# Blank TensorE products at the start of an attention and feed-forward kernel, and another order of its first loads

## The reference

```python
B, H, S, D = 4, 8, 576, 64
q_rot, k_rot = rotate(q), rotate(k)            # x1*cos - x2*sin, x1*sin + x2*cos on the halves of D
scores = matmul(q_rot, k_rot^T) / sqrt(D)      # per batch and head, 576 x 576
attn = exp(scores - max) / (sum + 1e-9)
x = (attn @ v), heads side by side             # 2304 tokens x 512
h = x @ w_in                                   # 2304 x 2048
g = max(h, 0) + alpha * min(h, 0)
out = g @ w_out                                # 2304 x 512
```

## Time and profile before

| | us |
|---|---|
| median of 3 runs | 696.17 |
| the profiled execution, whole | 695.67 |
| its span, first to last instruction | 693.9 |
| TensorE busy (PE) | 676.6 (98%) |
| VectorE busy | 369.5 (53%) |
| ScalarE busy | 316.6 (46%) |
| GpSimd busy | 281.9 (41%) |
| one queue's transfers, share of 16 DMA engines | 29.2% |

### The profile page before, as it was taken

One profiled execution on the slowest core, in us unless ns is written; L12 is line 12 of the kernel. 1 busy time (PEld: TensorE's weight loads), 2 busy tenths in 40 slices (PEclk: granted clock), 3 DMA queues, 4 the chain that ended last, 5 costly groups with the idle time before them and its releaser, 6 DMA issues.

```text
span 693.9 us, 12120 instructions
## 1 busy us (share of the span) xinstructions
PE 676.6 (98%) x4100; PEld 588.2 (85%) x4100; DVE 369.5 (53%) x681; ACT 316.6 (46%) x746; POOL 281.9 (41%) x260
## 2 busy tenths in 40 slices
PE   3899999999999999999999999999999999999998
PEld 3788888888888887698889999999999999999996
DVE  4688888888888887545642333333224322333222
ACT  2777777777777776433333222322222232223223
POOL 6655777777776503222222222222222222222222
PEclk9999999999999999999999999999999999999999
DMA  6898655666666643600001000000000000001001
GB/s 159 219 223 204 146 136 137 139 143 142 143 142 145 144 109 100 243 1 1 0 1 46 0 1 16 32 0 1 21 24 0 0 30 15 0 0 46 1 1 46
DMA packets 76619, 51.30 MB, mean 74 GB/s; under 512 B 61088, under 2 KB 61472, under 8 KB 76064
## 3 DMA queue, kind: packets, MB, share of 16 engines
q1 hardware_dynamic: 76576, 50.76, 29.2%
HBM read 22.95 MB, written 4.72 MB: 40 GB/s over the span
## 4 chain that ended last, share of the span: by engine, by line
PE 95%; DVE 2%; SPq 1%; DMA 1%; issue 0%; ACT 0%; POOL 0%; DVEq 0%
PE banks L635 29%; PE banks L664 29%; PE banks L559 14%; PE banks L517 11%; PE banks L581 10%; PE banks L577 2%; DMA k_two<-k_hi 1%; SPq L306 0%; DVE nmax L875 0%; DMA raw_q<-in_q 0%; SPq L307 0%; DVE pt L924 0%; SPq L291 0%; DVE prob L1044 0%; SPq L309 0%
## 5 line engine op out<-in xcount | busy, mean ns | idle before, releaser
L461 POOL TENSOR_TENSOR g_lo<-g,g_hi 128x384 fp32r<-128x384 f32 (+1 forms) x98 | 99.8, 1018 | 308.9 <-ACT g_hi L825 305.6
L990 DVE TENSOR_SCALAR g<-banks,alpha_sb 128x384 f32<-128x384 f32 (+1 forms) x98 | 59.8, 610 | 250.9 <-ACT pos L816 250.9
L635 PE MATMUL banks<-x_hi,w_in_lo 128*128 128x384 f32 x384 | 129.3, 337 | 0.0
L635 PE MATMUL banks<-x_hi,w_in_hi 128*128 128x384 f32 x384 | 129.2, 337 | 0.0
L635 PE MATMUL banks<-x_lo,w_in_hi 128*128 128x384 f32 x384 | 129.0, 336 | 0.0
L816 ACT ACTIVATE pos<-banks 128x384 f32<-128x384 f32 x96 | 47.1, 491 | 170.2 <-PE banks L635 170.2
L875 DVE TENSOR_REDUCE nmax<-banks 128x1 f32<-128x576 f32 x144 | 108.6, 755 | 25.2 <-PE banks L517 19.8
L664 PE MATMUL banks<-w_out_hi,g_hi 128*128 128x512 f32 x288 | 114.8, 399 | 0.3
L664 PE MATMUL banks<-w_out_hi,g_lo 128*128 128x512 f32 x288 | 112.9, 392 | 0.0
L664 PE MATMUL banks<-w_out_lo,g_hi 128*128 128x512 f32 x288 | 111.9, 389 | 0.0
L825 ACT ACTIVATE g_hi<-g 128x384 fp32r<-128x384 f32 (+1 forms) x98 | 50.9, 519 | 116.0 <-DVE g L993 116.0
(11 more groups left out here) (85 smaller groups left out, 907.4 us busy)
## 6 DMA issues: line engine op xcount, KB each, us to landing
k_two<-k_hi SPq DMA_DIRECT2D x64, 160.0 KB, 2.9
out<-stage SPq DMA_DIRECT2D x18, 256.0 KB, 2.0
raw_q<-in_q SPq DMA_DIRECT2D x32, 128.0 KB, 2.7
raw_k<-in_k SPq DMA_DIRECT2D x32, 128.0 KB, 2.4
q_two<-q_hi SPq DMA_DIRECT2D x32, 128.0 KB, 2.3
q_two<-q_lo SPq DMA_DIRECT2D x32, 128.0 KB, 2.3
q_own<-q_hi SPq DMA_DIRECT2D x32, 128.0 KB, 2.4
raw_v<-in_v SPq DMA_DIRECT2D x32, 128.0 KB, 2.3
```

What stands on the lines that cost most here:

```text
L461: nc.gpsimd.tensor_tensor(g_lo[f % 2][:, part], g[f % 2][:, part], g_hi[f % 2][:, part].bitcast(F32), ALU.subtract).then_inc(g_lo_done, 1)
L635: mm = nc.tensor.matmul(h_ps[f % 2], w[:, j, cols], xx[:, j, :], start=(step == 0), stop=(step == 3 * CT - 1))
L990: nc.vector.tensor_scalar(g[f % 2][:, part], h_ps[f % 2][:, part], 0.0, alpha_sb[:, f:f + 1], ALU.min, ALU.mult).then_inc(neg_done, 1)
```

## The change

- A new zeroed tile `blank` (128 x 128, float32), filled by VectorE, and `run_in(count)`: `count` products of `blank` with itself into PSUM bank 7, whose results nothing reads.
- 16 of these before the first transposes on TensorE, 4 between the transposes of q and of k of pair 0, 6 behind the last of them, and one ahead of each of the tiles 2 to 8 of period 0.
- `FIRST_TILES` holds tile 3 too, which then takes six products on 64 rows; tile 4 is the first that waits for the stacks. The high part of the next q waits for tile 3's products.
- ScalarE's queue issues the sin table and two of the four copies of the first k stack; the SyncE queue keeps the other two.
- In period 0 the order of SyncE's issues becomes: raw q of pair 2, q stack and k stack of pair 1, v of pair 0, raw k of pair 2.
- In period 0 the transposes of `U_K` and `U_MIXED` move behind tile 5's products; ScalarE takes tile 4's exponential ahead of the high parts of k, VectorE tile 5's maximum ahead of the low parts.
- VectorE and ScalarE wait for fewer of GpSimd's zero fills at the start.

```diff
-FIRST_TILES = (1, 2)
+FIRST_TILES = (1, 2, 3)
...
-            sp.dma_start(sin_sb[:, :, :], sin).then_inc(sin_in, 16)
             load(0, 0)
...
             stack(0, 0, 0)
-            stack(0, 0, 1)
+            sp.wait_ge(evac[U_K % T_BANKS], evac_count(-1, U_K))
+            sp.wait_ge(evac[U_MIXED % T_BANKS], evac_count(-1, U_MIXED))
+            for head, own in ((0, slice(0, D)), (1, slice(D, P))):
+                sp.dma_start(k_two[0][own, head, :].bitcast(F32), k_hi[0][own, :].bitcast(F32)).then_inc(k_two_in, 16)
...
                     if has_pair(p + 2):
                         load(p + 2, 0)
-                    load_v(b, t)
-                    if has_pair(p + 2):
+                    if not is_opening(p):
+                        load_v(b, t)
+                    if has_pair(p + 2) and not is_opening(p):
                         load(p + 2, 1)
                     if has_pair(p + 1):
                         stack(p + 1, (t + 1) % 2, 0)
                         stack(p + 1, (t + 1) % 2, 1)
+                    if is_opening(p):
+                        load_v(b, t)
+                        load(p + 2, 1)
...
+            def run_in(count):
+
+                for _ in range(count):
+                    nc.tensor.matmul(banks[:, 7, 0:P], blank[:, :], blank[:, :], start=True, stop=True)
+
             def score(p, t, n):
 
                 if not has_now(p):
                     return
+                if is_opening(p) and n > 1:
+                    run_in(1)
...
                 score(p, t, A_TILES[2])
-                turn(p, t, U_K)
-                turn(p, t, U_MIXED)
+                if not is_opening(p):
+                    turn(p, t, U_K)
+                    turn(p, t, U_MIXED)
...
                 score(p, t, B_TILES[0])
+                if is_opening(p):
+                    turn(p, t, U_K)
+                    turn(p, t, U_MIXED)
...
+            pe.wait_ge(blank_done, 1)
+            run_in(16)
             pe.wait_ge(ident_in, 16)
-            for u in (*OF_NEXT, U_MIXED):
-                turn(-1, -1, u)
+            turn(-1, -1, U_Q)
+            run_in(4)
+            turn(-1, -1, U_K)
+            turn(-1, -1, U_MIXED)
+            run_in(6)
...
+                    if isinstance(p, int) and p == 0:
+                        act.wait_ge(scored, FIRST_TILES[-1] + 1)
...
                 exps(p, t, A_TILES[2])
+                if is_opening(p):
+                    exps(p, t, A_TILES[3])
                 hi(p, U_K, t)
                 hi(p, U_MIXED, t)
-                exps(p, t, A_TILES[3])
+                if not is_opening(p):
+                    exps(p, t, A_TILES[3])
...
-            act.wait_ge(padded, PADDED)
+            act.dma_start(sin_sb[:, :, :], sin).then_inc(sin_in, 16)
+            act.wait_ge(padded, 4)
...
+            for own, head, other in ((slice(0, D), 0, slice(D, P)), (slice(D, P), 1, slice(0, D))):
+                act.dma_start(k_two[0][other, head, :].bitcast(F32), k_hi[0][own, :].bitcast(F32)).then_inc(k_two_in, 16)
...
+                if is_opening(p):
+                    maxima(p, t, B_TILES[0])
                 lo(p, U_K, t)
                 lo(p, U_MIXED, t)
...
-            nc.vector.memset(zero[:, :], 0.0).then_inc(padded, 1)
-            dve.wait_ge(padded, PADDED)
+            nc.vector.memset(blank[:, :], 0.0).then_inc(blank_done, 1)
+            nc.vector.memset(zero[:, :], 0.0).then_inc(blank_done, 1)
+            dve.wait_ge(padded, 2)
```

More of the change, by code:

```diff
@@ L50, in build @@
     PERIODS = NB * PAIRS
-    PADDED = 15
+    PADDED = 14
     W_COLS = F // (2 * PAIRS)
@@ L174, in build @@
             zero = sb(att, "zero", [P, 1])
+            blank = sb(att, "blank", [P, P])
         attention_bytes, used[0] = used[0], 0
@@ L220, in build @@
         first_step = sem("first_step")
+        blank_done = sem("blank_done")
         q_two_in, k_two_in = sem("q_two_in"), sem("k_two_in")
@@ L266, in chunks, with is_opening @@
             chunk(NCHUNK // 2 - 1, 1)
+        def is_opening(p):
+            return isinstance(p, int) and p == 0
         def is_first(i, c):
@@ L426, in _ @@
             pool.wait_ge(padded, PADDED)
+            pool.wait_ge(blank_done, 2)
             pool.wait_ge(sin_in, 16)
@@ L843, in _ @@
                 hi(-1, u, -1)
+            act.wait_ge(evac[U_K % T_BANKS], evac_count(-1, U_K))
+            act.wait_ge(evac[U_MIXED % T_BANKS], evac_count(-1, U_MIXED))
+            for own, head, other in ((slice(0, D), 0, slice(D, P)), (slice(D, P), 1, slice(0, D))):
+                act.dma_start(k_two[0][other, head, :].bitcast(F32), k_hi[0][own, :].bitcast(F32)).then_inc(k_two_in, 16)
             def batch(b):
@@ L1021, in period @@
                         split_x(0, 0, j)
-                maxima(p, t, B_TILES[0])
+                if not is_opening(p):
+                    maxima(p, t, B_TILES[0])
                 maxima(p, t, B_TILES[1])
```

## The result

The changed kernel takes 699.56 us (median of 5 runs, 698.65 to 701.77), the kernel before 696.17 (5 runs, 695.79 to 696.30): a ratio of 1.0060, 95% interval 1.0049 to 1.0071. It is slower by 3.4 us. The profiled execution took 701.77, with a span of 700.0 against 693.9.

A forecast was written before the change was run, and what follows sets the result against it. TensorE's order and waits bound the kernel, dense from 46 us. Transposes of k in period 1 move from 35.92 to 36.6, +0.7 us, kept to the end: median 696.17 becomes 696.9, range 695.2 to 700.4.

The forecast's parts named there:

- the rival with the fallen clock: Period 1, TensorE's new stall: clock falls to the low rate, 3 us lost over the 0.7, 699.9 us; chance 0.28.
- Part 1: Kernel start: raw q comes about 0.4 us earlier without the sin table on SyncE's queue; tile 0 starts 0.9 us earlier.
- Part 2: Blanks at the start and in period 0: 0.24 to 0.48 us each at the low rate, cost counted zero, clock likely raised.
- Part 4: Period 0, second k stack: issued at once when low parts of k are done at 23.15, landing at 28.1, not 31.90.
- Part 3: Period 0, tile 4: starts when the first k stack lands, taken as 18.5 us, between 17.75 and 19.0.
- E: Period 0: time when the second pair's high and low parts of k are done, 18.5 + 4.66 = 23.15 us.
- Part 5: Raw k of pair 2 behind stacks and v: rotated 13.44 us after the low parts, at 36.6; TensorE stands 4.5 us.
- The faster case: Period 1: raw k of pair 2 lands early, stall overrated, worth 3.8 us at best; chance 0.14.

The follow-up runs named there:

- The first k stack by SyncE alone: Changed kernel with raw k of pair 2 ahead of the stacks, all four first k stack copies back on SyncE's queue: 695.21 us, ratio 0.9974.
- the first experiment: Changed kernel with the SyncE queue's old order in period 0, blanks and new start kept: 697.33 us, ratio 1.0017.
- the third experiment: Changed kernel with raw k of pair 2 issued ahead of both stacks, only v left behind them: 694.13 us, ratio 0.9970.

## Why the prediction came out as it did

It forecast a small loss, 0.7 us, by a stall ahead of the transposes of k, and gave 0.28 to a clock that falls in it. The place, the mechanism and the sign were right; the forecast time of 696.9 was 2.7 us too low. The time was that of the rival with the fallen clock, 699.9 against 699.56, but by luck and not by its own sum: the shift that the stall leaves was 2.9 to 3.5 us in the two profiled executions and not 0.7, and the clock cost 1.6 to 2.5 and not 3. Luck is also that the five runs lie well inside the range of 695.2 to 700.4: the median of all ten is 700.40, at its upper edge.

- **Part 1, the start: wrong.** Raw q went out 0.4 us earlier, but landed 3.12 us after its last issue instead of 2.39, so at 4.94, 0.33 later than before. Tile 0 started at 12.87, not 12.1; what it won on 13.07 came from the quicker transposes. No run undid the move of the sin table alone, so that this move slowed raw q is not shown.
- **Part 2, the blanks: right but for one price.** 0.42 us a blank at the low rate lies inside the bounds of 0.24 and 0.48. They raised the clock, and products stayed at 0.13 us through period 0. Counted at zero, they came with an issue of the SyncE queue that took 1.82 us instead of 0.60 and delayed the second k stack (Part 4).
- **Part 3, the first k stack: right at the upper end, by other terms.** Tile 4 started at 19.23, so the stack landed at 19.1; the sum took 18.5 and named 19.0 as what the busy DMA engines would make of it. That 19.0 held 0.4 us of an earlier start, which were not there, and nothing for the sharing, which was worth 0.7 ("The first k stack by SyncE alone", 19.78 against 19.06). *The Trainium skill ("DMA: Bandwidth & Descriptors", Issuing engines are not separate DMA queues) says that a second issuing engine saves issue time only; the traces agree, with 0.7 us of landing out of 1.3 us of issue time.*
- **Part 4, the second k stack: failed.** The low parts were ready at 23.55 (E, forecast 23.15), but the stack wasn't "issued at once". It was first issued at 24.95, because the q stack ahead of it started at 19.93, not near 19, and needed 4.9 us: six issues, the last of which took 1.82 us instead of 0.60. The sum had asked only whether the q stack could start early, not when it would end. Cost: 1.8 us on everything behind, from 23.15 to 24.95. Of these 0.4 are the later low parts, 0.2 the q stack at its usual pace and 1.2 the one long issue, which nothing in the trace of before announced for this stretch.
- **Part 5, what is late next: the mechanism right, a term too small.** From the k stack's first issue to raw k's last it is 31.06 - 24.95 = 6.11 us, forecast 6.06. The landing took 3.42 us, where 2.54 had been taken (3.18 was the upper end). The rotation took 4.77, forecast 4.84, and 0.14 passed until TensorE started. Together with Part 4 the forecast of 36.6 falls short by 2.86 us of 39.46.
- **The fallen clock: right as a mechanism, too dear as a price.** The mean granted clock was 0.995 or 0.997 in all ten runs. The profiled executions lost 2.5 and 1.6 us by it; 3 had been taken. *The Trainium skill's warning of idle gaps ("TensorE: Matmul & The Clock Gate", Why this matters for your kernels) holds here: behind 5.47 and 4.79 us of standing both profiles show the low rate.*
- **The faster case** was refused for the right reason: TensorE was dense from 30 us to its stall, and then stood for raw k. The experiment with raw k ahead of the stacks shows that the second k stack's gain is real, 1.85 us of it, once raw k is no longer behind it.

## What to carry to other kernels

When a load is moved behind other work on a queue that issues in order, add up the issue times of all that now stands ahead of it, from the moment the queue is free and not from the moment the data is ready, and then its landing and its reader's whole chain. Put behind only what has slack: here v had it, while raw k had 5.5 us of slack (rotated at 30.46, read at 35.92) and came 9 us later. Warming products need the waits behind them covered too, or a faster start only reaches a longer wait, in which the clock is lost again.

## What the runs showed that was not expected

- The clock can fall behind a wait of 2.87 us, or of 2.41 (raw k ahead of v), and after the work has taken up again: in the first experiment the products at 32.08 ran at the high rate and those at 34.94 at the low one.
- The kernel before is not free of it. Of its 92 runs made beside the experiments, 80 had a mean granted clock of 0.999 or 1.000 and a median of 696.0 us; 12 had 0.995 to 0.998 and took 698.89 to 700.45, median 699.2. That is 3.2 us, close to the 3 that the prediction had taken for a fall. Where in these runs the clock falls is open, as no profile of one was kept.
- The granted clock that the profile prints is 1.00 for the first 23 us of the kernel before, where products ran 0.24 us apart; the later fall, after a rise, is printed as 0.50.
- One issue of the SyncE queue between 22.7 and 25.5 us took 1.1 to 2.2 us instead of 0.6 in all ten profiled kernels with blanks, whichever transfer it was, and none did in the four without (the one before, the new order alone, raw k first in the kernel before, and raw k first without blanks). The last differs from the third experiment by the blanks only. It costs the second k stack 0.5 to 1.6 us.
- In all fourteen profiles such a long issue goes with a transfer of another kind, a load of instructions (`q8 instruction`): between 22.7 and 24 us with blanks, and between 32.2 and 35.5 without, where the kernel before has an issue of 1.67 us at 35.23. The two lines are from 23 to 24 us of the changed kernel and from 35 to 36 us of the one before:

```profile
q8 instruction: 1, 0.02, 7.9%
...
q8 instruction: 1, 0.02, 7.5%
```

  When it came, TensorE had 120 recorded products behind it in the changed kernel (a blank counts as two) and 122 in the one before, while VectorE had 25 instructions against 37 and ScalarE 23 against 42. So it seems to follow TensorE's instructions, and the blanks bring it forward into the q stack's issues. That this load is what holds the issue up is not shown: other issues of 1.0 to 1.8 us, such as one of 1.34 at 33.84 in the kernel before, have no such load beside them.
- A product of 128 x 128 zeros in float32 takes 0.42 us at the low rate and 0.23 at the high one (20 of them in 4.63 us), and zeros raise the clock and keep it.
